# Moving one subtraction of the second feed-forward stage from VectorE to GpSimd

## What is computed

```python
h = np.maximum(x @ w_in, 0.0)
conv_out = sum(conv_w[k] * hp[:, k:k + S, :] for k in range(3))   # hp is h padded by one token
gate = 1.0 / (1.0 + np.exp(-conv_out))
return h * gate @ w_out
```

## Time and profile before

| what | value |
|---|---|
| median of three runs | 557.43 us (557.41 to 557.67) |
| profiled execution | 556.83 us, its span 554.6 us |
| second stage in the span | 347 us to the end |
| VectorE busy | 344.1 us, 62% of the span |
| ScalarE busy | 283.8 us, 51% |
| GpSimd busy | 133.1 us, 24%; nothing after 358.7 us |

### The profile page before, as it was taken

How to read it: one execution, slowest core, us unless ns; L and a number is a source line. 1 busy time by engine, 2 the same in 40 slices (tenths; PEclk the granted TensorE clock), 3 DMA queues, 4 the chain that set the end, 5 groups by cost and what they waited for, 6 DMA issues and landing times.

```text
span 554.6 us, 15245 instructions
## 1 busy us (share of the span) xinstructions
PE 538.9 (97%) x6171; PEld 490.2 (88%) x6174; DVE 344.1 (62%) x864; ACT 283.8 (51%) x773; POOL 133.1 (24%) x157
## 2 busy tenths in 40 slices
PE   8589999999999999999999999999999999999997
PEld 4357899999999999999999999997898799889976
DVE  5465896767667676586575571997088218815920
ACT  3319829549259177087194260293176127516721
POOL 8036993204013013022032187800000000000000
PEclk9879999999999999999999999999999999999999
DMA  9767424223234133044100705300300130010011
GB/s 217 117 142 202 75 72 66 60 69 62 47 73 72 33 85 69 22 97 80 44 4 6 277 1 152 129 2 38 124 2 0 58 123 0 0 57 19 0 38 57
DMA packets 99443, 38.67 MB, mean 70 GB/s; under 512 B 92596, under 2 KB 92616, under 8 KB 99380
## 3 DMA queue, kind: packets, MB, share of 16 engines
q1 hardware_dynamic: 93908, 27.45, 21.1%
q0 software_dynamic: 2496, 7.66, 4.2%
q10 hardware_dynamic: 2976, 2.69, 2.0%
HBM read 28.33 MB, written 9.44 MB: 68 GB/s over the span
## 4 chain that ended last, share of the span: by engine, by line
PE 81%; SPq 6%; DVE 5%; ACT 2%; issue 2%; POOL 2%; DMA 2%; ACTq 0%
PE ps L677 16%; PE ps L667 14%; PE ps L567 9%; PE ps L568 8%; PE ps L569 8%; PE ps L618 6%; PE ps L619 6%; PE ps L620 6%; SPq L269 5%; PE ps L481 3%; PE ps L524 3%; DVE cbuf L1102 2%; PE ps L512 2%; POOL wb_lo L412 1%; DMA wv_raw<-in_moe_w_v_dram 1%
## 5 line engine op out<-in xcount | busy, mean ns | idle before, releaser
L420 POOL TENSOR_TENSOR k_lo<-k,k_hi 128x288 fp32r<-128x288 f32 x64 | 58.7, 921 | 187.3 <-ACT k_hi L729 187.1
L1102 DVE SCALAR_TENSOR_TENSOR cbuf<-hbuf,cols_c,cbuf 128x576 f32<-128x576 f32 x64 | 56.4, 883 | 61.1 <-ACT cbuf L818 59.9
L618 PE MATMUL ps<-k_hi,wb_hi 128*128 128x288 f32 x256 | 75.6, 295 | 0.2 <-POOL wb_lo L412 0.2
L619 PE MATMUL ps<-k_lo,wb_hi 128*128 128x288 f32 x256 | 75.5, 295 | 0.0
L620 PE MATMUL ps<-k_hi,wb_lo 128*128 128x288 f32 x256 | 75.4, 295 | 0.0
L567 PE MATMUL ps<-xk_hi,wa_hi 128*128 128x288 f32 x224 | 68.4, 305 | 0.0
L569 PE MATMUL ps<-xk_hi,wa_lo 128*128 128x288 f32 x224 | 66.1, 295 | 0.0
L568 PE MATMUL ps<-xk_lo,wa_hi 128*128 128x288 f32 x224 | 66.1, 295 | 0.0
L677 PE MATMUL ps<-wb_hi,g_hi 128*128 128x512 f32 x144 | 57.7, 401 | 0.4 <-DVE g_lo L1117 0.2
L677 PE MATMUL ps<-wb_hi,g_lo 128*128 128x512 f32 x144 | 56.9, 395 | 0.0
L677 PE MATMUL ps<-wb_lo,g_hi 128*128 128x512 f32 x144 | 56.5, 393 | 0.0
(11 more groups left out here) (106 smaller groups left out, 1239.9 us busy)
## 6 DMA issues: line engine op xcount, KB each, us to landing
x2d<-x2s SPq DMA_DIRECT2D x8, 576.0 KB, 3.1
x2raw<-x2d SPq DMA_DIRECT2D x4, 1152.0 KB, 5.4
out_dram<-ob SPq DMA_DIRECT2D x16, 256.0 KB, 2.0
raw<-in_q_dram SPq DMA_DIRECT2D x112, 36.0 KB, 2.1
raw<-in_k_dram SPq DMA_DIRECT2D x112, 36.0 KB, 2.0
vl<-in_v_dram SPq DMA_DIRECT2D x32, 72.0 KB, 2.1
wk_raw<-in_moe_w_k_dram ACTq DMA_DIRECT2D x4, 512.0 KB, 10.4
wv_raw<-in_moe_w_v_dram POOLq DMA_DIRECT2D x4, 512.0 KB, 8.2
```

The source lines that it names most:

```text
L420: nc.gpsimd.tensor_tensor(k2_lo[:, m], k2[:, m % K2RING], k2_hi[:, m].bitcast(F32), ALU.subtract).then_inc(k2_done, 1)
L618: nc.tensor.matmul(dst, wb_hi[:, f, cols], k2_hi[:, f, :], start=(f == 0), stop=False)
L619: nc.tensor.matmul(dst, wb_hi[:, f, cols], k2_lo[:, f, :], start=False, stop=False)
L1102: nc.vector.scalar_tensor_tensor(out=c, in0=h[:, o:o + S], scalar=conv[:, o, m:m + 1], in1=c, op0=ALU.mult, op1=ALU.add).then_inc(conv_ste ...
```

## The change

`lower` goes from VectorE's list to GpSimd's, behind all that GpSimd did, as a loop over pairs of batches with 16 subtractions in each pass. The operands, the shapes (128x576) and the semaphores are the same. VectorE's loop over tiles is one step shorter.

```diff
@@ GpSimd @@
                 low_w2(i)
                 if i + WRING < W2:
                     load_w2(i + WRING)
+
+            def lower(b, e, m):
+                wait(pool, g_hi_done, FT * (b + 1) + m + 1)
+                toks = slice(REST * e, REST * e + S)
+                nc.gpsimd.tensor_tensor(g_lo[:, m, toks], gf[:, m % GRING], g_hi[:, m, toks].bitcast(F32),
+                                        ALU.subtract).then_inc(g_lo_done, 1)
+
+            with pool.Fori(0, B // 2) as pair:
+                for e in range(2):
+                    for m in range(FT):
+                        lower(2 * pair + e, e, m)
@@ VectorE @@
-                def lower(m):
-                    wait(dve, g_hi_done, FT * (b + 1) + m + 1)
-                    toks = slice(REST * e, REST * e + S)
-                    nc.vector.tensor_tensor(g_lo[:, m, toks], gf[:, m % GRING], g_hi[:, m, toks].bitcast(F32),
-                                            ALU.subtract).then_inc(g_lo_done, 1)
-
-                for m in range(FT + 2):
+                for m in range(FT + 1):
                     if m < FT:
                         convolve(m)
-                    if m >= 2:
-                        lower(m - 2)
-                    if 1 <= m <= FT:
+                    if m >= 1:
                         apply_gate(m - 1)
                 if not last:
                     split_x2(b + 1)
```

## The result

The changed kernel takes 575.7 us (median of six runs, 574.62 to 577.6) against 557.42 us (six runs, 556.87 to 557.67): 1.0334 times as long, 95% interval 1.0322 to 1.0345. The forecast was 571.6 us, range 563 to 578. The profiled execution took 575.03 us, its span is 573.2 us, 18.6 us longer than before.

The account below looks back on a forecast made before the run. TensorE, busy 97% of the span, was taken as the bound. Batch delays 6.6 + 3.7 + 3.7 + 0.2 = 14.2 us on 556.83 gave 571.0, plus 0.6 to the median: 571.6 us, range 563 to 578.

Parts of the forecast that it names:

- VectorE's relief is worth nothing: Second stage: VectorE loses 21 us of busy time, worth nothing except about 0.4 us of TensorE's old wait.
- 1.43 us for a subtraction of 128x576: GpSimd's time alone for each moved subtraction, taken from a line between measured sizes; bounds 1.36 and 1.61 us.
- The two exclude each other and take turns; period 3.48 us: VectorE and GpSimd block each other for whole instructions; VectorE's tile period goes from 2.92 to 3.48 us, above TensorE's 3.19.
- Two signs: Signs of being right: GpSimd's new rows' median well above 1.43 us; line 1102 or 1111 mean 0.6 to 1.2 us higher.
- the narrow one: Rule that only VectorE's two-port instructions and GpSimd's block each other, sparing taps and gate; by it, time about 557.0 us.
- Tail: cast, g_lo(6), x_lo, g_lo(7): Order at the end of the first three batches: split_x2's cast and x_lo (2.40 us) delay GpSimd's last two subtractions.
- A gentler tail: Rival: g_lo(7) gets in ahead of x_lo, saving about 2.4 us in each of three batches: 564.4 us; chance 0.16.
- The sum by batch: Added time in the four batches' output products: 6.6 + 3.7 + 3.7 + 0.2 = 14.2 us.
- The clock at 1.00 after 380 us: Sign for TensorE: a granted clock below 1.00 after 380 us would show the prediction wrong.
- the room in the second batch: Slack before TensorE needs g_lo of tile 7 at 431.26: up to 1.6 us later costs nothing.
- a rival with 0.15: TensorE's waits drop its clock to 1.2 GHz, each fall losing up to 3.4 us: 575 to 578 us; chance 0.15.

## Why the prediction was right

The mechanism held: exclusion, a period longer than TensorE's, and the order in the tail. The size came out 4 us short, the turn in the period was taken in another place than worked out, and one of the signs named for being wrong did come.

- *VectorE's relief is worth nothing.* Right. The run that fills with zeros puts the whole of it at 0.9 us.
- *1.43 us for a subtraction of 128x576.* The undisturbed ones measure 1.43.
- *The two exclude each other and take turns; period 3.48 us.* Measured 3.50, but not by the steps worked out. The prediction puts the subtraction between the taps and the gate, held by the taps and ending 1.28 us after them. In the trace it falls between the two taps and is not held, since g_hi comes just as the first tap ends; the second tap waits. What it adds is the same, 2.90 - 1.67 = 1.23 us, so the period came out right. Two signs failed for it: the median of GpSimd's new rows is 1.430 us and not well above 1.43, and the taps have a mean 0.39 us above before (1.269 against 0.883), the gates 0.15 (0.904 against 0.752), not 0.6 to 1.2, as only one tap of each pair is held.
- *Which instructions conflict.* Of the two rules in view the narrow one, that only VectorE's two-port instructions conflict with GpSimd's (the one that the prediction takes from the Trainium skill, Advanced Engine Details and Errata, Mode Summary), is refuted by the taps of every run that subtracts. The Trainium skill (SBUF — State Buffer, SBUF: two separate sides) has the wider one: a VectorE instruction with two SBUF inputs also excludes GpSimd's, but only one that reads SBUF. The runs agree on both halves: 1.27 us a tap against the subtraction, 0.82 against the filling.
- *Tail: cast, g_lo(6), x_lo, g_lo(7).* Right in the first three batches, and shown as cause by three runs that take it apart. "A gentler tail", which I gave 0.16, did not come.
- *The sum by batch*, from TensorE's first output matmul to that of tile 7 (of tile 6 in the fourth), against before: 390.66 - 373.72 is 16.94 against 10.14, +6.8 (forecast 6.6); 443.09 - 429.17 is 13.92 against 9.81, +4.1 (3.7); the third the same (3.7); 549.96 - 540.87 is 9.09 against 8.41, +0.7 (0.2). Together 15.7 against 14.2.
- *The clock at 1.00 after 380 us.* Wrong. A granted clock below it was named as a sign of being wrong, and it fell to 0.53 behind the second batch's waits.

**Terms mis-sized.** First, the 1.5 us in the sum by batch: 0.2 in the first batch, 0.4 to 0.5 in each of the others. TensorE begins with tile 7 0.05 us after g_lo(7) is there, whatever stops it made before. Some 0.16 of each later batch is a misreading of the earlier trace rows: 421.45 is where the chain changes its line, and the output product's first matmul had begun before that, in TensorE's timeline of the kernel before:

```profile
421.29 0.40 PE L677 MATMUL ps<-wb_hi,g_hi 128*128 128x512 f32 x1
...
431.09 0.40 PE L677 MATMUL ps<-wb_hi,g_hi 128*128 128x512 f32 x1
```

So g_lo of tile 7 was wanted at 431.1, not at 431.26, and the room in the second batch was 1.4 us, not 1.6. The rest is g_lo(7) itself: it ends at 443.04, 13.87 us after the first output matmul, where the prediction has 434.9 - 421.29 = 13.61.

Second, the restarts, a term that the prediction does not have. Behind a stop the second matmul follows the first after 0.34 us instead of 0.23; with it, the output products of the second to fourth batches lose 0.1 each beyond the sum above, 0.35 in all.

Third, the clock. I had it as a rival with 0.15 beside the forecast; it is an addition to it, 1.2 us in the profiled run, and the slower unprofiled runs, at a lower mean clock, may have more. The median, 575.7, does lie in the 575 to 578 that this rival had named, but one fall costs 1.2 us and not the up to 3.4 us that it was priced at.

Fourth, 1.1 us of the profiled span lie before the stage (its first matmul at 348.2 against 347.1), and 0.2 in the stage's first products (25.5 us each, where two of the four took 25.4 before). The other profiles, with the same first stage, begin the stage anywhere from 347.3 to 348.8, so it need not come from the change; the cause stays open. 15.7 + 0.35 + 1.2 + 1.1 + 0.2 = 18.55 of the span's 18.6.

## What to carry to other kernels

As these runs show it, an elementwise instruction moved from VectorE to GpSimd takes VectorE's time anyway if both read SBUF and VectorE's have two inputs there: count the longer GpSimd duration into VectorE's stream, and compare the new period with that of the bounding engine. Then look for the long VectorE instruction that stands next in line when the last, urgent one on GpSimd is due; a wait that holds back work nobody needs yet took back two thirds of the loss here. Even so, no variant that subtracts on GpSimd was faster than the kernel before. And a bounding engine that begins to stop pays for each restart (0.1 us here) and may lose its clock (1.2 us for one fall here).

## What the runs showed that I had not expected

GpSimd's filling, 0.58 us with no input, leaves two-input VectorE instructions alone (x_lo 2.56 us) but not the one-input cast between SBUF tensors (1.80 against 1.35 us). And TensorE's granted clock fell behind waits of 1.5 to 3.0 us with six full matmuls between them, though not in every batch nor in the same one in every run: in the second batch of the changed kernel's profile (waits of 1.70 and 2.00 us), in the first of the run where only x_lo waits (1.5 and 3.0 us), and in neither the first nor the third of the changed kernel's, whose waits are as long.
